# Pooled attention scores issued as pairs of heads on TensorE's two row halves

## What is computed

```python
# 1: pooled attention (4 tokens to 1, 144 left) + local attention (|i - j| < 4)
q_d, k_d, v_d = (a.reshape(B, H, 144, 4, D).mean(axis=3) for a in (q, k, v))
out_up = np.repeat(sm_attn(q_d, k_d, v_d), 4, axis=2)
scores = np.where(mask, scale * q @ k.T, -1e9); out_local = softmax(scores) @ v
x = out_up + out_local
# 2: real part of a 2-d Fourier transform, layer norm, a two-layer MLP of 2048
u = x + real(fft(fft(x, axis=1), axis=2)); un = layer_norm(u)
x = u + relu(un @ w_ch1) @ w_ch2
# 3: a gate from a causal convolution of 5 taps, and two projections
out = sigmoid(conv5(x)) * (x @ w_val) @ w_out
```

## Time and profile before

| what | value |
|---|---|
| time, median of 3 runs | 814.59 us (813.22 to 815.72) |
| the profiled execution: its own time | 811.06 us |
| the profiled execution: span, first to last instruction | 809.2 us |
| PE busy | 737.7 us (91%) |
| PE weight loads busy | 546.8 us (68%) |
| DVE busy | 403.7 us (50%) |
| ACT busy | 191.8 us (24%) |
| POOL busy | 148.8 us (18%) |
| share of the chain that ended last: PE, POOL, DVE, SP's queue | 68%, 10%, 7%, 5% |
| mean granted clock of PE | 0.979 |

### The profile page before, as it was taken

One profiled execution on the slowest core, in us unless ns is written; L12 is line 12 of the kernel. 1 busy time (PEld: TensorE's weight loads), 2 busy tenths in 40 slices (PEclk: granted clock), 3 DMA queues, 4 the chain that ended last, 5 costly groups with the idle time before them and its releaser, 6 DMA issues.

```text
span 809.2 us, 15617 instructions
## 1 busy us (share of the span) xinstructions
PE 737.7 (91%) x5960; PEld 546.8 (68%) x5960; DVE 403.7 (50%) x927; ACT 191.8 (24%) x417; POOL 148.8 (18%) x126
## 2 busy tenths in 40 slices
PE   1779755989999998999999998999999999999998
PEld 1555343777776776777776776787776777777776
DVE  3437276743653684643643684743643780113552
ACT  1336431222221212222221223222212122111101
POOL 7105569980100210000100210000100300000000
PEclk9999956999999999999999999999999999999999
DMA  9875046213100004513101105413100000000001
GB/s 292 239 171 175 25 137 156 49 29 77 28 1 31 31 30 138 98 29 75 30 1 31 31 29 151 85 29 79 25 2 1 1 29 30 2 1 1 2 15 45
DMA packets 42106, 49.15 MB, mean 61 GB/s; under 512 B 4784, under 2 KB 35568, under 8 KB 40944
## 3 DMA queue, kind: packets, MB, share of 16 engines
q1 hardware_dynamic: 33392, 31.69, 16.4%
q10 hardware_dynamic: 8640, 16.43, 5.9%
HBM read 43.38 MB, written 4.72 MB: 59 GB/s over the span
## 4 chain that ended last, share of the span: by engine, by line
PE 68%; POOL 10%; DVE 7%; SPq 5%; issue 4%; DMA 3%; ACT 1%; ACTq 0%; DVEq 0%; POOLq 0%
PE P L539 20%; PE Y L556 20%; PE P L668 4%; PE Y L657 4%; PE A L565 3%; PE Y L668 3%; SPq L416 3%; POOL w L1322 3%; POOL w L1326 2%; PE A L526 2%; PE A L519 2%; PE A L618 1%; SPq L408 1%; PE A L607 1%; PE A L462 1%
## 5 line engine op out<-in xcount | busy, mean ns | idle before, releaser
L539 PE MATMUL P<-unT,w_wv 128*128 128x288 f16 x1536 | 213.3, 290 | 10.3 <-DVE hT L1095 5.0
L556 PE MATMUL Y<-hT,w 128*128 128x288 f16 x1536 | 215.0, 286 | 3.9 <-POOL w L1328 2.4
L1095 DVE SCALAR_TENSOR_TENSOR hT<-P,hT 128x288 f16<-128x288 f32 x128 | 58.4, 457 | 263.0 <-ACT hT L779 263.0
L539 PEld LDWEIGHTS P<-unT,w_wv 128*128 128x128 f16 x1536 | 149.7, 99 | 55.7 <-issue 12.0
L556 PEld LDWEIGHTS Y<-hT,w 128*128 128x128 f16 x1536 | 144.8, 98 | 48.3 <-issue 9.6
L779 ACT ACTIVATE hT<-P 128x288 f16<-128x288 f32 x128 | 52.6, 411 | 198.9 <-PE P L539 198.8
L1131 DVE SCALAR_TENSOR_TENSOR gate<-xT,cw,gate 128x288 f32<-128x288 f32 x128 | 66.4, 519 | 4.5
L750 ACT ACTIVATE prob_or_un<-prob_or_un 73x288 f32<-73x288 f32 (+1 forms) x52 | 23.3, 448 | 128.7 <-DVE prob_or_un L968 128.7
L1261 POOL MEMSET x<- 1x512 f32 x4 | 2.1, 516 | 228.5 <-ACT x L768 228.5
L565 PE MATMUL A<-sdft,pair_or_folded 128*128 128x289 f32 (+5 forms) x102 | 32.8, 444 | 4.6 <-DVE pair_or_folded L1025 4.6
L297 POOL TENSOR_TENSOR x<-x,fb 128x256 f32<-128x256 f32 (+1 forms) x12 | 11.8, 987 | 116.7 <-DVE fb L1036 116.7
(11 more groups left out here) (169 smaller groups left out, 894.2 us busy)
## 6 DMA issues: line engine op xcount, KB each, us to landing
kl<-qk_win SPq DMA_DIRECT2D x38, 140.0 KB, 4.2
ql<-qk_win SPq DMA_DIRECT2D x19, 256.0 KB, 3.8
vl<-v_win SPq DMA_DIRECT2D x72, 65.0 KB
pair_or_folded<-qk_pool SPq DMA_DIRECT2D x8, 580.0 KB, 5.7
pair_or_spectrum<-qk_pool SPq DMA_DIRECT2D x8, 580.0 KB, 7.1
out<-ot ACTq DMA_DIRECT2D x32, 144.0 KB, 1.8
w_wv<-w_ch ACTq DMA_DIRECT2D x4, 1024.0 KB, 11.9
w<-w_ch ACTq DMA_DIRECT2D x4, 1024.0 KB, 6.6
```

The source lines that it names most:

```text
L539: last = mm(P[s % 2][:, 0:HN], w1s(k, f, wt), unT[:, ut, k, ha * HN:(ha + 1) * HN], start=k == 0 and wt + ut == 0, stop=k == KD - 1 and wt ...
L556: last = mm(Y[d][:, 0:HN], w2s(f, d, wt), hT[s % 3][:, ht, :], start=f == 0 and wt + ht == 0, stop=f == KF - 1 and wt == 1)
L1095: nc.vector.scalar_tensor_tensor(out=hT[s % 3][:, 1, :], in0=P[s % 2][:, 0:HN], scalar=0.0, in1=hT[s % 3][:, 0, :], op0=ALU.max, op1=ALU.s ...
```

## The change

Heads are taken in pairs, (0, 1), (2, 3), (4, 5), (6, 7), one pair in every second slot: 2, 4, 6, 8. `pair_scores` issues the four score matmuls of a pair in turn on rows 0 to 63 and 64 to 127, into banks A[0] and A[1]. The two transposes come one slot later, one ahead of the first part of `mlp_down` and one between its parts, and the two products with the values at the end of that slot, together. A pair's scores wait until both heads of the pair before are normalised (`normed`), which DVE does in the odd slot. Local tiles move by one slot, to 10, 12, 14, 16, 18, and with them the folds. `pool_v(b, 1)` moves from slot 2 to slot 1. The opening takes pairs too: at even s two transposes, a pair's scores, two products.

```diff
@@ -236,11 +236,11 @@
         UD = H
         SLOTS = 2 * KF
         S0 = 1
-        SCORES_AT = [S0 + u for u in range(UD)] + [S0 + UD + 2 * i for i in range(NT)]
+        SCORES_AT = [2 + u for u in range(UD)] + [2 + UD + 2 * i for i in range(NT)]
         LAG_SCALE, LAG_T, LAG_AV, LAG_DOWN = 1, 2, 3, 2
         CONV_AT = [22, 24, 26, 28]
 
-        POOLING = {2: [("v", 1)], 3: [("qk", 2)], 5: [("qk", 3)]}
+        POOLING = {1: [("v", 1)], 3: [("qk", 2)], 5: [("qk", 3)]}
         POOLING_FIRST = {1: [("qk", 1)], 3: [("qk", 2)], 5: [("qk", 3)]}
         WEIGHT_LOADS = {1: [0], 2: [1], 3: [2], 4: [3], 7: [4], 8: [5], 13: [8, 6], 14: [7]}
         SQUARES = {4: 0, 5: 1, 6: 2, 7: 3, 8: 4, 9: 5, 10: 6, 11: 7, 12: 8, 13: 9, 14: 10, 15: 11}
@@ -260,6 +260,8 @@
 
             if opening(b):
                 return Y[u % 2], Y[2 + u % 2], P[u % 2]
+            if u < UD:
+                return A[u % 2], A[u % 2], A[u % 2]
             return A[0], A[1], A[1]
 
         def values(b, t):
@@ -284,7 +286,11 @@
 
             if m is None:
                 return [s - S0 - lag] if 0 <= s - S0 - lag < NU else []
-            return [u for u in range(NU) if b is not None and SCORES_AT[u] + lag == s]
+            return [u for u in range(UD, NU) if b is not None and SCORES_AT[u] + lag == s]
+
+        def pair_at(b, s, lag):
+
+            return [u for u in range(0, UD, 2) if b is not None and SCORES_AT[u] + lag == s]
 
         def mixed_banks(b, j):
 
@@ -430,6 +436,23 @@
         def _(pe):
             mm = nc.tensor.matmul
 
+            def pair_scores(b, u):
+
+                n = b * NU + u
+                if opening(b) and u >= 2:
+                    pe.wait_ge(shifted, n)
+                elif u >= 2:
+                    pe.wait_ge(normed, UD * b + u)
+                elif later(b):
+                    pe.wait_ge(uT_sb, 6 * b)
+                pe.wait_ge(qk_pooled, b * 4 + u // 2 + 1)
+                for t in range(2):
+                    for h in range(2):
+                        qk = qkd[D * h:D * h + D, u // 2, :]
+                        last = mm(banks(b, u + h)[0][0:GQ, t * G:(t + 1) * G], qk[:, t * GQ:(t + 1) * GQ], qk[:, 2 * GQ:GT], start=True, stop=True)
+                        if t == 1:
+                            last.then_inc(scores, 1)
+
             def unit_scores(b, u):
                 n = b * NU + u
 
@@ -437,30 +460,22 @@
                 if later(read):
                     pe.wait_ge(shifted, read)
                 S = banks(b, u)[0]
-                if u == 0 and later(b):
-                    pe.wait_ge(uT_sb, 6 * b)
-                if u < UD:
-                    r0 = D * (u % 2)
-                    if u % 2 == 0:
-                        pe.wait_ge(qk_pooled, b * 4 + u // 2 + 1)
-                    qk = qkd[r0:r0 + D, u // 2, :]
-                    for t in range(2):
-                        last = mm(S[0:GQ, t * G:(t + 1) * G], qk[:, t * GQ:(t + 1) * GQ], qk[:, 2 * GQ:GT], start=True, stop=True)
-                else:
-                    t = u - UD
-                    if opening(b) and t == 0:
...
+                if u == UD and not opening(b):
+                    pe.wait_ge(normed, UD * (b + 1))
+                t = u - UD
...
 
             def unit_transpose(b, u):
@@ -472,9 +487,9 @@
                 if not opening(b):
                     if u == 0:
                         pe.wait_ge(x_sb, NT * b)
-                    elif u <= UD:
+                    elif u == UD:
                         pe.wait_ge(normed, UD * b + u)
-                    else:
+                    elif u > UD:
                         pe.wait_ge(x_sb, NT * b + u - UD)
                 elif u >= 2:
                     pe.wait_ge(probT_done, n - 1)
@@ -674,26 +689,40 @@
                     for s in range(NU + LAG_T):
                         if s == W1_AT:
                             weight_sum(0)
-                        if s >= LAG_T:
-                            if s == LAG_T:
-                                pe.wait_ge(ld_id, 16)
-                            unit_transpose(b, s - LAG_T)
-                        if s < NU:
+                        if s == LAG_T:
+                            pe.wait_ge(ld_id, 16)
+                        done = [s - 2, s - 1] if s % 2 == 0 and LAG_T <= s <= UD else [s - LAG_T] if s >= UD + LAG_T else []
+                        for u in done:
+                            unit_transpose(b, u)
+                        if s < UD and s % 2 == 0:
+                            pair_scores(b, s)
+                        elif UD <= s < NU and s != UD + 1:
                             unit_scores(b, s)
-                        if s >= LAG_T:
-                            unit_av(b, s - LAG_T)
+                            if s == UD:
+                                unit_scores(b, s + 1)
+                        for u in done:
+                            unit_av(b, u)
                 for s in range(SLOTS + LAG_DOWN if m is not None else 0):
                     down = s >= LAG_DOWN
                     if s < SLOTS:
                         mlp_up(m, s)
                     for u in unit_at(b, m, s, LAG_AV):
                         unit_av(b, u)
+                    for u in pair_at(b, s, 1):
+                        unit_transpose(b, u)
                     if down:
                         mlp_down(m, s - LAG_DOWN, 0)
                     for u in unit_at(b, m, s, 0):
                         unit_scores(b, u)
+                    for u in pair_at(b, s, 0):
+                        pair_scores(b, u)
+                    for u in pair_at(b, s, 1):
+                        unit_transpose(b, u + 1)
                     if down:
                         mlp_down(m, s - LAG_DOWN, 1)
+                    for u in pair_at(b, s, 1):
+                        unit_av(b, u)
+                        unit_av(b, u + 1)
                     for u in unit_at(b, m, s, LAG_T):
                         unit_transpose(b, u)
                     if b is not None:
@@ -877,6 +906,12 @@
                     for u in unit_at(b, m, s, 0):
                         unit_exp(b, u)
                     if m is not None:
+                        for u in pair_at(b, s, 0):
+                            unit_exp(b, u)
+                            unit_exp(b, u + 1)
+                        for u in pair_at(b, s, 1):
+                            unit_probT(b, u)
+                            unit_probT(b, u + 1)
                         for u in unit_at(b, m, s, LAG_T):
                             unit_probT(b, u)
                     for u in unit_at(b, m, s, LAG_AV):
@@ -1155,11 +1190,27 @@
                     if m is not None and s == KF + LAG_DOWN:
                         residual(m, 0)
                     if b is not None:
-                        for u in unit_at(b, m, s, LAG_AV):
-                            if u < UD:
+                        first = s - S0 if m is None else -1
+                        if 0 <= first < UD and first % 2 == 0:
+                            unit_shift(b, first)
+                            unit_shift(b, first + 1)
+                            if first >= 2:
+                                unit_norm(b, first - 2)
+                                unit_norm(b, first - 1)
+                        if first == UD:
+                            unit_shift(b, UD)
+                            unit_norm(b, UD - 2)
+                            unit_norm(b, UD - 1)
+                        for u in unit_at(b, m, s, 0):
+                            if u > UD or m is not None:
+                                unit_shift(b, u)
+                        if m is not None:
+                            for u in pair_at(b, s, 0):
+                                unit_shift(b, u)
+                                unit_shift(b, u + 1)
+                            for u in pair_at(b, s, 1):
                                 unit_norm(b, u)
-                        for u in unit_at(b, m, s, 0):
-                            unit_shift(b, u)
+                                unit_norm(b, u + 1)
                         for u in unit_at(b, m, s, LAG_SCALE):
                             if u >= UD:
                                 unit_scale(b, u)

```

More of the change, by code:

```diff
@@ L439, in unit_scores @@
                 S = banks(b, u)[0]
-                if u == 0 and later(b):
-                    pe.wait_ge(uT_sb, 6 * b)
-                if u < UD:
-                    r0 = D * (u % 2)
-                    if u % 2 == 0:
-                        pe.wait_ge(qk_pooled, b * 4 + u // 2 + 1)
-                    qk = qkd[r0:r0 + D, u // 2, :]
-                    for t in range(2):
-                        last = mm(S[0:GQ, t * G:(t + 1) * G], qk[:, t * GQ:(t + 1) * GQ], qk[:, 2 * GQ:GT], start=True, stop=True)
-                else:
-                    t = u - UD
-                    if opening(b) and t == 0:
-                        pe.wait_ge(ld_const, CONSTS)
-                    QL, KL, landed, count = keys(b, t)
```

(26 more changed lines are left out.)

## The result

The change makes the kernel slower: 824.36 us against 814.59 us (medians of five runs each, 820.89 to 828.5 and 812.14 to 815.72), a ratio of 1.013 with an interval of 1.008 to 1.017. Timed again later, it was 824.79 against 812.37 us, 1.014 (1.012 to 1.017). The forecast was 825.5 us.

What follows compares the result with a forecast made beforehand. PE's own list was taken to set the pace. Opening +0.5 and iterations +3.1, +3.0 and +4.2 us made +10.8 us on the 814.6 us median, 825.4, rounded to 825.5 us; eight in ten 818 to 832 us.

Steps and rivals of the forecast that it cites:

- stall ahead of the first transpose: Slot 3, iterations 2 and 3: PE waits for the exponential behind the moved pooling, 3.9 and 5.6 us.
- four steps named: Start of iteration 3: pooling, hidden_low, a shift and the exponential precede the first transpose, 5.43 us together.
- residual's wait: Slot 18 of each iteration: mlp_down waits, no local tile's value product hiding it; +1.5 us each, +4.5 us in all.
- (b): Rival: the row halves don't overlap in the loop, 0.75 us more per pair at most; 833.5 us, chance 0.10.
- (c): Rival: the transfer for pool_v(b, 1) is there when DVE comes to it; 815.6 us, no change, chance 0.08.
- (d): Rival: faster, beyond (c) the residual is hidden too; 811.1 us, chance 0.04.
- The pairs' saving: Head slots in the loop: a pair's scores cost what one head's did, 0.8 us saved per pair, 3.2 us per iteration.
- The clock: Behind the stalls of iterations 1, 2 and 3: matmuls run slowly after idleness, 1.6 us each, +4.8 us.
- old stall: Pooling's wait ahead of the first value product goes away: 0.59 us (iteration 2), 1.08 (iteration 3), about 0.2 late restart each.
- Rival (a): The stalls come but the clock stays up: 820.7 us, chance 0.13.
- Iteration 1: Pairs gain nothing because mlp_down(8) waits for POOL, about 6.1 instead of 2.40 us; with clock and residual +3.1 us.
- The opening: Ahead of the loop: nothing to gain before a load's wait of 2.82 us; +0.5 us, from 0 to +2.5.

Runs made afterwards that it cites:

- second profile: The changed kernel run and profiled once more with nothing altered: 824.79 us, ratio 1.014 to the kernel before.
- both slots mended: Changed kernel with pool_v(b, 1) back in slot 2 and local tiles' scores from slot 11: 812.11 us, ratio 0.997 to the kernel before.

## Why the prediction was right, and where its sum was off

**Time, sign and the two chief causes: right.** The stall ahead of the first transpose is there, from the late transfer through the four steps named: 4.73 and 5.36 us against 3.9 and 5.6 (in the second profile 5.14 and 4.62). The transpose starts 14.7 and 13.6 us into iterations 2 and 3 where 13.7 was forecast for both. The residual's wait of 1.42 us stands in each iteration, 1.5 forecast, and undoing it gave 5.5 us for 4.5. Rivals (b), (c) and (d) are out: the halves overlap, and DVE did wait for the transfer, 3.3 to 3.9 us each time in the first profile and 2.5 to 4.3 in the second.

**The pairs' saving: right in size**, 0.72 us a pair, 2.9 us an iteration instead of 3.2; the 0.1 us that the two products together might have saved is not there.

**The clock: the term that was mis-sized.** "1.6 us each" behind a stall, taken from two rows of idleness ahead of long runs of matmuls. It measured 4.6 and 4.5 us in the first profile and 2.4 and 4.7 in the second. In the worst of them nearly all that follows the stall, up to 10 us of it, runs at the lower level (1.2 GHz) before the rate returns. It is tempting to blame the kind of work there (blocks of 6 matmuls, transposes, value products), but in two other kernels (both heads on one half, heads not in turn) the same blocks lost 1.7 us three times, about what was forecast. So 1.6 us is the low end of a range that two rows couldn't show, and what picks the value in it is not shown by any run here. With the measured sizes the sum closes: iteration 2: -2.9 + 4.7 - 0.6 + 1.4 + 4.6 = 7.2 of 7.7 us; iteration 3: -2.9 + 5.4 - 1.1 + 1.4 + 4.5 = 7.3 of 7.4 us (pairs, stall, old stall, residual, clock). The Trainium skill (TensorE: Matmul & The Clock Gate, Terms) puts the penalty of throttled time at half of that time, for a clock at half rate; an estimate by it is 4.9 us for 9.8 us at the lower level, and the trace, with 4.5, roughly agrees. Rival (a), a clock that stays up, came true only in iteration 1: behind the transposes' stall of 1.61 us in the second profile, and behind POOL's wait of 2.12 us in the first.

**The clock at the start of an iteration was not in the sum.** I read the length of the idleness there as what decides (2.46 us: loss, 2.13: none). It is not. The first matmuls of iterations 2 and 3 in the timeline of the changed kernel's first profile:

```profile
320.14 6.25 PE L554 MATMUL P<-unT,w_wv 128*128 128x288 f16 x36 [3.13 <-issue]
...
509.14 4.58 PE L554 MATMUL P<-unT,w_wv 128*128 128x288 f16 x36 [2.45 <-issue]
```

and in that of its second:

```profile
322.20 3.11 PE L554 MATMUL P<-unT,w_wv 128*128 128x288 f16 x24 [2.65 <-issue]
...
507.90 6.25 PE L554 MATMUL P<-unT,w_wv 128*128 128x288 f16 x36 [2.03 <-issue]
```

36 take 4.58 us at the full rate and 6.25 where the first of them are slow; 24 take 3.11 at the full rate. 3.13 and 2.03 us of idleness were followed by the slow rate, 2.45 and 2.65 by the fast one. It moves 1.7 us an iteration between executions. Before, iteration 2 began slowly and iteration 3 fast, and so they did in the first profile after; in the second it was the other way round, which takes iteration 2 to -2.9 + 5.1 - 0.6 + 1.4 + 2.4 - 1.7 = 3.7 of 4.4 us, and iteration 3 to -2.9 + 4.6 - 1.1 + 1.4 + 4.7 + 1.7 = 8.4 of 8.6 us.

**Iteration 1: right in its bound, wrong in its parts.** From its first `mlp_up` to `mlp_down(8)` it took 51.99 us before and 52.01 after, in both profiles: the pairs save nothing as long as POOL's chain ends there. But I had all of PE's spare time in the wait for POOL (6.1 us). The transfer of v took 9.9 us there (issued at 130.05, DVE on at 139.93), so 2.90 or 1.61 us went into the same stall of the transpose and 2.12 or 5.04 us into POOL's. Of the loss behind, +2.4 and +4.4 us, 1.4 are the residual's and about 0.4 the different blocks that follow. The rest is 0.7 us of longer idleness ahead of iteration 2 in the first profile (3.13 instead of 2.46 us), where no matmul behind POOL's wait was slow, and in the second 2.5 us of slow matmuls behind POOL's 5.04 us. So the clock's 1.6 us of this iteration was nothing in one profile and 2.5 in the other.

**The opening: the sign was wrong, and it is small.** +0.5 us forecast, -1.0 measured; of that 0.9 us are matmuls that reached the full rate earlier at 92 us (2 in 0.67 us and 4 in 1.33, where before they took 1.17 and 1.68), which is no work of the pairs, and the other three kernels with the old opening lie at 126.5, 126.9 and 127.0 us. So what the pairs gain in the opening can't be told from chance.

**Why the median was right while the sum was short** of the profiled pair can only be bounded: the runs of the changed kernel spread over 7.6 us, and both profiled ones lie some 3 us above its median, the profiled one of before 3.5 us under its own. The clock's chance can make most of that: the kernel with the heads not in turn does the same work, and its profiled execution, 820.44 us, lost 1.7 us behind each of its stalls instead of up to 4.7. That it is what happened in the runs without a profile wasn't shown. So the close agreement of 825.5 with 824.36 us is in part luck: with the 3.4 us that the clock cost on average behind the stalls of iterations 2 and 3 in place of 1.6, the same sum gives some 829 us.

## What to carry to other kernels

Before an operation is moved ahead of another on an engine, list all that is queued behind it and which of it frees a bank: the pooling's move cost 6 us even without the pairs, through a bank that I hadn't looked at. Price a stall on TensorE twice, for itself and for the slow stretch behind it, and give the second a range: two rows elsewhere gave 1.6 us, ten cases of this stall 1.7 to 4.7. And when a change saves time ahead of a wait for another engine, mend that wait first: the same pairs, with both slots mended, were worth 0.3% with the old wait for the weight chunks and 0.8% without it.

## What the runs showed of the hardware

Four fp32 matmuls of 64 rows and 144 columns take 0.72 us on two row halves and 1.20 us on one, 1.67 times as long, in whatever order they are issued. Behind stalls of 3.0 to 5.4 us the same blocks of matmuls and transposes took 7.0 to 10.1 us instead of 5.3, in ten cases of ten, and the longer stall was not always the dearer one; 60 matmuls of 216 columns in its place (5.71 us) kept the full rate in both cases. And the same kernel, at the same place, behind 2.0 to 3.1 us of idleness, starts at either rate: idleness of that length doesn't settle which.
